# One core, LSH attention and two mixture-of-experts layers: row loads issued ahead of the stores, tile tables made earlier, tile numbers read once, 20 dummy products

## The reference

```python
def reference(**kwargs):
    attn_out = _attn_ref(q, k, v, proj)          # B 2, H 8, S 768, D 64; a query sees keys of its own hash bucket
    x = attn_out.transpose(0, 2, 1, 3).reshape(1536, 512)
    x = _moe_ref(x, w_gate, w_noise, noise, w1, w2)      # top 2 of 8 experts
    return _moe2_ref(x, w_gate2, w1_2, w2_2)             # top 1 of 8 experts

# in _moe_ref, for every expert e and every choice k (D 512, F 1024):
    mask = top2[:, k] == e
    h = np.maximum(x[mask] @ w1[e], 0.0)
    out[mask] += top2_w[mask, k, None] * (h @ w2[e])
```

## Time and profile before

| | us |
|---|---|
| median of 3 runs (lowest, highest) | 969.62 (969.14, 972.87) |
| profiled execution | 968.24 |
| its span, first to last instruction | 966.5 |
| attention, to about | 296 |
| routing of layer 1, to the first `up` | 327.1 |
| wide stage, first `up` to last `down_rows` | 327.1 to 705.4 |
| mean granted clock of TensorE, share of full | 0.951 |

### The profile page before, as it was taken

The page is one execution under the profiler, slowest core; times in us unless marked ns, Lnnn a source line. Parts: engine busy times, 40 slices in busy tenths (PEclk is TensorE's granted clock), DMA queues, the critical chain, the costliest instruction groups (busy, mean ns, idle before and its releaser), DMA issues.

```text
span 966.5 us, 15853 instructions
## 1 busy us (share of the span) xinstructions
PE 832.0 (86%) x4770; PEld 749.0 (77%) x4771; DVE 559.9 (58%) x997; ACT 373.5 (39%) x625; POOL 400.6 (41%) x294
## 2 busy tenths in 40 slices
PE   3899999999985655989989899989696899999991
PEld 2788888888874545979989898989475788888871
DVE  4899999999976443435244444524047644445540
ACT  1778787878873011112221111210341334333003
POOL 2010110101222764333454433434624899895204
PEclk9999999999997677999999999999877999999996
DMA  6577659666896564334453533431767878784107
GB/s 148 127 208 219 166 150 239 185 146 185 233 347 210 204 203 151 110 134 121 142 171 107 191 109 135 126 127 60 219 205 264 275 246 258 232 261 163 43 33 272
DMA packets 100214, 172.14 MB, mean 178 GB/s; under 512 B 35600, under 2 KB 37648, under 8 KB 100160
## 3 DMA queue, kind: packets, MB, share of 16 engines
q1 hardware_dynamic: 65088, 79.35, 27.9%
q10 hardware_dynamic: 28672, 71.05, 23.1%
q0 software_dynamic: 6400, 20.98, 6.5%
HBM read 97.36 MB, written 54.53 MB: 157 GB/s over the span
## 4 chain that ended last, share of the span: by engine, by line
PE 70%; DMA 9%; DVE 8%; issue 6%; another core or an unknown queue 2%; SPq 2%; ACT 2%; POOL 1%; POOLq 1%; ACTq 0%; DVEq 0%
PE bank L1451 7%; PE bank L1710 4%; PE bank L1712 4%; PE bank L1711 4%; DMA ys<-work 3%; PE bank L1724 3%; PE bank L1725 3%; PE bank L1726 3%; DMA work<-xs 3%; PE bank L1439 3%; PE bank L1462 3%; PE bank L1621 3%; PE bank L1463 3%; PE bank L1622 3%; PE bank L1623 3%
## 5 line engine op out<-in xcount | busy, mean ns | idle before, releaser
L636 POOL TENSOR_TENSOR wring<-stage,wring 128x1024 fp32r<-128x1024 f32 (+1 forms) x116 | 274.2, 2396 | 196.6 <-ACT wring L840 182.9
L840 ACT ACTIVATE wring<-stage 128x1024 fp32r<-128x1024 f32 (+1 forms) x116 | 121.0, 1059 | 388.4 <-PE bank L1726 114.2
L1710 PE MATMUL bank<-wring 128*128 128x400 f32 x256 | 93.1, 364 | 9.8 <-DVE wring L1339 7.8
L758 ACT ACTIVATE wring<-bank 128x384 fp32r<-128x384 f32 x192 | 84.2, 493 | 38.2 <-PE bank L1451 38.1
L987 DVE TENSOR_TENSOR wring<-bank,wring 128x768 fp32r<-128x768 f32 x96 | 91.9, 958 | 12.1 <-ACT wring L758 10.2
L748 ACT ACTIVATE work<-bank,stat 128x768 f32<-128x768 f32 x96 | 95.5, 995 | 8.0 <-DVE stat L981 6.4
L1724 PE MATMUL bank<-wring 128*128 128x400 f32 x224 | 80.2, 358 | 21.2 <-issue 14.7
L622 POOL TENSOR_TENSOR rinv<-rsum,least_sum 128x6 f32<-128x6 f32 x16 | 3.1, 196 | 227.3 <-ACT work L748 227.3
L978 DVE TENSOR_REDUCE stat<-bank 128x1 f32<-128x768 f32 x96 | 91.5, 953 | 8.0 <-PE bank L1440 6.0
L1712 PE MATMUL bank<-wring 128*128 128x400 f32 x256 | 90.5, 354 | 0.7 <-issue 0.7
L1451 PE MATMUL bank<-ident,work 128*128 128x128 f32 x576 | 81.4, 278 | 11.0 <-DVE wring L987 6.1
(11 more groups left out here) (217 smaller groups left out, 1765.4 us busy)
## 6 DMA issues: line engine op xcount, KB each, us to landing
stage<-in_moe_w_dram ACTq DMA_DIRECT2D x128, 512.0 KB, 4.3
wring<-wring SPq DMA_DIRECT2D x92, 192.0 KB
ys<-work SPq DMA_DIRECT2D x40, 256.0 KB
xs<-stage SPq DMA_DIRECT2D x7, 768.0 KB, 4.4
ys<-stage SPq DMA_DIRECT2D x7, 768.0 KB, 5.8
work<-xs SPq DMA_DIRECT2D x7, 768.0 KB, 4.7
xs<-stage SPq DMA_DIRECT2D x7, 512.0 KB, 6.6
ys<-stage SPq DMA_DIRECT2D x7, 512.0 KB, 6.6
```

The source lines that it names most:

```text
L636: nc.gpsimd.tensor_tensor(wring[:, bass.ds(at + DC * F, GW)], stage[:, at_stage(g, j), :], wring[:, bass.ds(at, GW)].bitcast(F32), ALU.sub ...
L840: nc.scalar.activation(wring[:, bass.ds(high_at(m, e, j), GW)], stage[:, j % STAGES, :], ACT.Copy).then_inc(w_high, 1)
L1710: mm(to, high, wide_x[0][:, c], start=c == 0, stop=False)
```

## The change

Row loads are issued one tile further ahead, in front of the stores (and one more than there are tiles, for which the tables get an entry more; POOL waits for the last of them before it overwrites `work`). `later_rows` and `tables(0)` stand before the first `x_split`. The last three pieces of the first tile are gathered one scatter earlier. PE reads all eight tile numbers and the last but one (`but_last`) after the first tile's blocks are turned, and its program is cut into tiles (`up`, `down`) rather than steps (`down`, `up`). 20 dummy products stand behind the first `turn_x`.

```diff
-        row_of = sb("row_of", [1, NT[0]], I32)
+        row_of = sb("row_of", [1, NT[0] + 1], I32)
+        but_last = sb("but_last", [1, 1], I32)
...
             wide_load(1)
+            wide_load(2)
             wide_store(0)
             with sp.Fori(2, NTMIN[0]) as t:
-                wide_load(t)
+                wide_load(t + 1)
                 wide_store(t - 1)
             with sp.Fori(NTMIN[0], NT[0]) as t:
                 with sp.If(used_wide > t):
-                    wide_load(t)
+                    wide_load(t + 1)
                     wide_store(t - 1)
...
-                fetch_at = ((1, 5, 5, 5), (1, 4, 5, 6))[m]
+                fetch_at = ((1, 4, 4, 4), (1, 4, 5, 6))[m]
...
                 for t in range(TT):
+                    if m == 0 and t == EARLY:
+                        loads = pool.value_load(tiles_upto[0][0:1, E - 1:E], min_val=NTMIN[0], max_val=NT[0])
+                        pool.wait_ge(wide_ld, loads * 32)
+                        pool.sem_inc(y_seen, 1)
...
+                    link(vec.tensor_scalar(but_last[:], cum[0:1, E - 1:E], -2.0, None, ALU.add))
...
+                later_rows(0)
+                tables(0)
                 for b in range(NB):
-                    if b == 1:
-                        later_rows(0)
                     x_split(0, b)
                 gate_weights(0)
                 for f in range(FC):
                     h_split(0, f)
                     if f < GRAN // 2:
                         low_by_vector(0, 0, GRAN // 2 + f)
-                tables(0)
                 dve.wait_ge(rt_tab, 1)
...
-                def step(t, e, before, e_before):
-                    pe.wait_ge(w_low, e_before * GRAN + GRAN)
...
+                def up_all(t, e, before):
+                    pe.wait_ge(w_low, e * GRAN + GRAN // 2)
+                    for f in range(FC):
+                        up(t, f, 2 * e % 3 * HALF_W)
+                        if f in BACK_AT and not at_start(t):
+                            turn_y(before, BACK_AT.index(f))
+
+                def tile(t, e, before):
+                    up_all(t, e, before)
+                    pe.wait_ge(w_low, e * GRAN + GRAN)
+                    for d in range(DC):
+                        down(t, d, (2 * e + 1) % 3 * HALF_W)
+                        if d < DC - 1:
+                            turn_x(t + 1, d)
+                        if d == DC - 2:
+                            turn_x(t + 1, d + 1)
+
                 for b in range(NB):
                     turn_x(0, b)
-                pe.wait_ge(w_low, GRAN // 2)
-                for f in range(FC):
-                    up(0, f, 0)
+                    if b == 0:
+                        keep_busy(20, wide_down[0][:, 0:P])
                 pe.wait_ge(rt_tab, 1)
...
+                finals = [last_tile(e) for e in range(E)]
+                before_final = pe.value_load(but_last[0:1, 0:1], min_val=E - 2, max_val=NT[0] - 2)
+                for e in range(E - 1):
+                    final = finals[e]
+                    if e == 0:
+                        tile(0, 0, None)
...
+                    else:
+                        before = finals[e - 1]
+                        tile(before + 1, e, before)
+                        with pe.If(final > before + 1):
...
+                final, before = finals[E - 1], finals[E - 2]
+                with pe.If(final > before + 1):
...
+                up_all(final, E - 1, before_final)
```

More of the change, by code:

```diff
@@ L1172, in tables @@
                 link(vec.tensor_copy(last_seen[0:1, TT - 1:TT], cnt[0:1, E - 1:E]))
-                nt = NT[m]
+                nt = NT[m] + (m == 0)
                 if m == 0:
@@ L1524, in _, with keep_busy @@
             turn_back(2 * H - 1, 1, H - 1)
-            def keep_busy(n):
+            def keep_busy(n, to=y_ps[:, 0:P]):
                 for i in range(n):
-                    mm(y_ps[:, 0:P], ones[:], ident[:], start=True, stop=True)
+                    mm(to, ones[:], ident[:], start=True, stop=True)
             def route(m):
@@ L1765, in step @@
                         up(t, f, 2 * e % 3 * HALF_W)
-                        if f in BACK_AT:
+                        if f in BACK_AT and not at_start(t):
                             turn_y(before, BACK_AT.index(f))
+                def tile(t, e, before):
[7 more added lines that the diff above has]
+                            turn_x(t + 1, d + 1)
                 for b in range(NB):
                     turn_x(0, b)
-                pe.wait_ge(w_low, GRAN // 2)
-                for f in range(FC):
-                    up(0, f, 0)
+                    if b == 0:
+                        keep_busy(20, wide_down[0][:, 0:P])
                 pe.wait_ge(rt_tab, 1)
-                for e in range(E):
-                    final = last_tile(e)
-                    if e:
-                        step(before + 1, e, before, e - 1)
+                finals = [last_tile(e) for e in range(E)]
[4 more added lines that the diff above has]
+                        tile(0, 0, None)
+                        with pe.If(final > 0):
+                            with pe.Fori(0, WIDE_MAX - 1) as i:
+                                with pe.If(final > i):
+                                    tile(i + 1, 0, i)
+                    else:
+                        before = finals[e - 1]
+                        tile(before + 1, e, before)
                         with pe.If(final > before + 1):
@@ L1781, in wide_experts @@
                                 with pe.If(final > before + i):
-                                    step(before + 1 + i, e, before + i, e)
-                    else:
-                        with pe.If(final > 0):
-                            with pe.Fori(0, WIDE_MAX - 1) as i:
-                                with pe.If(final > i):
-                                    step(i + 1, 0, i, 0)
-                    before = final
+                                    tile(before + 1 + i, e, before + i)
+                final, before = finals[E - 1], finals[E - 2]
+                with pe.If(final > before + 1):
+                    with pe.Fori(0, WIDE_MAX - 1) as i:
+                        with pe.If(before_final > before + i):
+                            tile(before + 1 + i, E - 1, before + i)
+                up_all(final, E - 1, before_final)
                 pe.wait_ge(w_low, E * GRAN)
                 for b in range(NB):
-                    down_rows(before, b, (2 * E - 1) % 3 * HALF_W)
+                    down_rows(final, b, (2 * E - 1) % 3 * HALF_W)
             route(0)
```

## The result

| | before | changed |
|---|---|---|
| median of 15 runs | 968.17 us | 953.09 us |
| lowest and highest | 959.65, 972.87 | 945.65, 958.27 |
| ratio | | 0.9846, 95% interval 0.9815 to 0.9877 |
| profiled execution | 968.24 | 955.44 |
| its span, granted clock | 966.5, 0.951 | 953.5, 0.946 |

The kernel is 15.1 us faster, where 25 were forecast. In the two profiled executions it is 13.0 us of span. A measured time moves by 13 us from run to run in both kernels, so differences of a few microseconds are read from intervals or from rows, not from single runs. Ratios leave out the few executions in which the core was in a slower state with a lower granted clock, while medians hold all of them, so a ratio can differ a little from that of the two medians.

The account below looks back on a forecast made before the run. PE, busy 86% of the span, was taken to bound the kernel, so gains come from its idle time. The terms -14.8, -11.7 and +1.5 sum to -25.0: 968.24 becomes 943.2, as a median 944.6, given as 944, range 931 to 957.

Parts of the forecast that it names:

- Tables early, -14.8: Before the first `down`: the 12.97 us gap goes whole, with 1.8 us of slow clock behind it; -14.8 us.
- Nine register loads, 0 by the cover: Ahead of the first `up`: it starts 2.3 to 5.1 us later, hidden by the 7.83 us wait within it; counted 0.
- the 357 to 365: Sign of being wrong: the first `up` ending outside this span in us; it was expected to end near 361.
- the stall in the first `up` goes: Rival, first `up`: the stall moves with DVE's program to where nobody waits; about -6 us, 938.5; chance 0.15.
- Dummies, 0: Ahead of the first `up`: 20 dummy products take at most 9.0 us, absorbed by the wait there; value 0, at most +1.
- Row loads ahead, -11.7: Before six of the seven later `turn_x`: PE's waits for row loads, 11.7 us in all, go; -11.7 us.
- about 350: Tile 1's row load: waits for the scatters alone, until about this time in us, ample for a `down` at 361.
- Tiles for steps, +1.5: Expert boundaries: 8.8 us go, seven new ones before an `up` cost 10.3 at 4.0 a branch; +1.5 (-5.7 to +4.2).
- Branches of 5 us and more: Sign of being wrong: PE's taken branches at the boundaries lasting this long, where 4.0 us was assumed.
- code is loaded behind the rows: Rival, seven boundaries: a branch's code waits for the whole row load, 5.0 us each, 35 more; 980 us; chance 0.05.

Follow-up runs that it names:

- the second profile: The changed kernel, unaltered, profiled again on another, slower chip beside that chip's own runs of the kernel before: 963.65 us, ratio 0.9885.

## Why the prediction was off by ten microseconds

*Tables early, -14.8: right.* The gap of 12.97 is gone and the tables run from 315.34 to 319.41 under the wait for the first rows. Alone the part measured 10.4 us by its ratio, with 7.3 us of grown row waits and 3.7 us of the gap left; the spans have 15.5, but only one of the two has VectorE's stalls.

*Nine register loads, 0 by the cover: size right, the cover a matter of the execution.* In the first profile the first `up` starts at 331.26, within 329.4 to 332.2. The cover, the 7.83 us wait, is missing, so 4.1 us are paid and 7.8 gained, and the `up` ends at 351.05, outside the 357 to 365 that I had named as a sign of being wrong. In the second profile the wait is there (7.1 us), and the `up` ends at 364.1, within it, though it had started only at 335.40. So the rival "the stall in the first `up` goes" came true in one execution by luck and not in the other. Neither is the change's doing. Why the stall comes in some executions is open.

*Dummies, 0: right.*

*Row loads ahead, -11.7: right for the six waits, one new wait missed.* Tile 1's load waits for the last scatter to land and is issued at 353.62, and `turn_x` waits 4.54 us for it. I had called "about 350" ample for a `down` at 361; without the stall that `down` begins at 350.9, and its first turn was due at 355.4. In the second profile, with the stall, the `down` begins at 364.0 and this wait doesn't occur.

*Tiles for steps, +1.5: this is the term that failed.* I took 4.0 us for a branch and 10.3 for the boundaries. They measured 5.65 and 21.7 us in both profiles, so +12.9 for +1.5. "Branches of 5 us and more" was the other sign of being wrong, and it came. In the first profile 9.0 us of slower matmuls in `up` come on top, for which the sum had no term; in the second they are 1.8. The groups of `up`, before and changed (busy us, mean ns), have 274.0 and 283.0 us:

```profile
L1710 PE MATMUL bank<-wring 128*128 128x400 f32 x256 | 93.1, 364 | 9.8 <-DVE wring L1339 7.8 <-issue 1.4 <-DVE hT_hl L1328 0.7
L1712 PE MATMUL bank<-wring 128*128 128x400 f32 x256 | 90.5, 354 | 0.7 <-issue 0.7
L1711 PE MATMUL bank<-hT_hl,wring 128*128 128x400 f32 x256 | 90.4, 353 | 0.0
```

```profile
L1716 PE MATMUL bank<-wring 128*128 128x400 f32 x256 | 96.7, 378 | 28.7 <-issue 28.7
L1717 PE MATMUL bank<-hT_hl,wring 128*128 128x400 f32 x256 | 93.4, 365 | 0.0
L1718 PE MATMUL bank<-wring 128*128 128x400 f32 x256 | 92.9, 363 | 0.0
```

Moving one transfer gives both back (0.9641 for 0.9846). The rival "code is loaded behind the rows" had the mechanism and the place right, with 2 us a branch and not 5. Its price of 5.0 was the load's time from issue to landing. The code did stand behind nearly the whole load, but that moved its packet only from 1.0 to 3.3 us behind the branch, since the load was issued ahead of the branch and its packets passed in some 2 us (417.0 to 419.0). I gave the rival 0.05 at the price of 5.0.

*What the sum left out behind the last tile.* `down_rows` is 12.6 us shorter in the first profile, its stalls missing, which the second profile shows to be the execution's doing and not the change's. The route and layer 2 give 9.6 back (5.6 + 4.0): with the route's turns at once behind it, PE waits 2.8 us for ScalarE's copy and runs five pairs of turn and logits at 2.45 us, as against three in the kernel before, and the granted clock is 0.76 for 0.85.

In one line, for the first profile, up to the start of `down_rows`: -14.8 - 11.7 + 12.9 + 9.0 + 4.5 + 4.1 - 7.8 = -3.8, and two small waits of before (1.35 and 1.22 us, ahead of 340.29 and 588.28) that are gone make it -6.4. Read are -9.95, so 3.6 us stay unplaced. With 12.6 more in `down_rows` and 9.6 given back the end is 13.0 earlier. The second profile, from the third chip, has no 4.5, 4.1 or 7.8, as the stalls are those of the kernel before: its first `down` starts 9.95 us earlier than before, 1.8 come from the clock there, 11.7 are gained and 12.9 paid, -10.6, and read are -10.4. Changed kernel and kernel before are then alike in their stalls, and the -25.0 with 11.4 more at the boundaries would be -13.6, against 15.1 measured in the medians. That sum is an estimate, but it says which term was off. The range held the time with errors that partly cancel.

## What to carry over

Ask of each taken branch on a busy engine which transfers are issued in the microsecond ahead of it: here the same load, moved some 12 us away, was worth 2% of the kernel, in two pairs of kernels. A gap on PE can cost more than its length, if the matmuls behind it run at the slow clock; 21.7 us of gaps and the slow matmuls made 34 us in one pair of profiles, but the same gaps came with 4.3 us less of PE's busy time in another execution. A wait that "covers" an added cost is only as good as its cause is known. And before a wait that is gone is put down to a change, profile the same kernel twice: here 7.1 and 8.9 us of waits came and went with no edit at all.

## What the runs showed of the hardware

- A taken branch on PE at a boundary takes 3.1 to 4.3 us with no row load just ahead of it on SyncE's queue (once 4.9, the first one with tables early), and 5.6 to 5.75 with one issued 0.66 us ahead (5.3 to 5.7 in the second profile, 5.88 once in the TensorE program of before). One record in six is 425 ns, though the gap behind it is 2.4 us like the others. The last of two branches in a row takes 4.6 to 6.1, and why 6.1 with the load moved away is open.
- Some small VectorE operations are held while GpSimd computes. The `CAST` of 1x8 above, 0.16 us elsewhere, took 9.91 us and ended with GpSimd's four low parts (348.32 + 9.23 = 357.55). In the kernel with row loads ahead alone, a `TENSOR_TENSOR` of 128x64 did the same:

```profile
347.56 9.65 DVE L1071 TENSOR_TENSOR raw<-raw,tri_in 128x64 f32<-128x64 f32 x1
...
347.90 9.23 POOL L637 TENSOR_TENSOR wring<-stage,wring 128x1024 fp32r<-128x1024 f32 x4
```

  The 2.04 us of the table operation in the earlier trace rows end at 364.36, and GpSimd's operations in that trace at 354.93 + 9.38 = 364.31. In the changed kernel, where GpSimd only issues scatters, the same operation takes 0.21. The Trainium skill (GPSIMD Engine Reference, section "1. Specifications") says that GpSimd's way into SBUF is shared with VectorE and contended by instructions with two SBUF inputs or in a two-port mode; the `TENSOR_TENSOR`s agree, and for the `CAST` no row tells its mode. No run varied this by itself.
- The load of a register from SBUF took 295 to 736 ns on PE, 448 in the median of eight in a row.
- In five of 14 profiles VectorE stands idle for 5 to 18 us at a time while GpSimd issues scatters or gathers, though its input has long been made (15.2 us until 349.49 and 17.5 until 684.89 in the second profile of the changed kernel). In the other nine, the changed kernel's first profile among them, it doesn't. The cause is open.
